# Three opening tiles rebuilt: a convolution summed on TensorE, halves copied by ScalarE and VectorE, GpSimd relieved, a growing lookahead

## What is computed

```python
# attention part: x (4, 4096, 192), weight_gen (4, 4096, 8 heads, 7 taps)
w = exp(weight_gen - max(weight_gen, -1)); w = w / (sum(w, -1) + 1e-9)
y[b, s, h, g] = sum_k w[b, s, h, k] * x_pad[b, s + k, h, g]      # 6 zeros of padding ahead
# layer: 16384 tokens, d_model 192, d_ff 1536
xn = y / sqrt(mean(y * y, -1) + 1e-6) * rms_g
g = xn @ w_gate; out = (g * sigmoid(g) * (xn @ w_val)) @ w_out
```

## Time and profile before

| quantity | us |
|---|---|
| median of 3 runs | 1334.81 |
| lowest, highest | 1332.93, 1335.38 |
| the profiled execution | 1334.78 |
| its span on the core | 1333.0 |

### The profile page before, as it was taken

How to read it: one execution, slowest core, us unless ns; L and a number is a source line. 1 busy time by engine, 2 the same in 40 slices (tenths; PEclk the granted TensorE clock), 3 DMA queues, 4 the chain that set the end, 5 groups by cost and what they waited for, 6 DMA issues and landing times.

```text
span 1333.0 us, 33644 instructions
## 1 busy us (share of the span) xinstructions
PE 1280.2 (96%) x13524; PEld 1230.0 (92%) x13524; DVE 995.2 (75%) x1438; ACT 662.8 (50%) x1427; POOL 97.1 (7%) x104
## 2 busy tenths in 40 slices
PE   3797899999999999999999999999999999999998
PEld 3686789999988889999999999999999999999998
DVE  6777867877777777777777777777777777777653
ACT  4364464455554455554445555445555544555543
POOL 7701200000000000000000000000000000000000
PEclk9798899999999999999999999999999999999999
DMA  9121111122112212212112211211221211121010
GB/s 306 35 67 25 50 58 55 37 67 67 49 60 64 57 37 66 66 43 66 54 40 63 66 58 51 66 55 37 66 66 43 66 55 52 52 66 34 16 37 13
DMA packets 20101, 77.69 MB, mean 58 GB/s; under 512 B 3215, under 2 KB 5007, under 8 KB 19854
## 3 DMA queue, kind: packets, MB, share of 16 engines
q1 hardware_dynamic: 19982, 75.83, 19.0%
HBM read 38.07 MB, written 12.58 MB: 38 GB/s over the span
## 4 chain that ended last, share of the span: by engine, by line
PE 91%; DVE 3%; ACT 2%; issue 2%; DMA 1%; POOL 0%; SPq 0%; POOLq 0%
PE up_ps L619 59%; PE out_ps L650 24%; PE out_ps L654 7%; DVE h L545 1%; DMA xT<-xT 1%; DVE prod L201 1%; PE up_ps L587 1%; DVE y L203 1%; ACT silu L422 0%; DVE tap_max L522 0%; ACT taps L403 0%; DVE h_lo L565 0%; ACT xn L386 0%; PE up_ps L591 0%; DMA taps<-in_weight_gen 0%
## 5 line engine op out<-in xcount | busy, mean ns | idle before, releaser
L619 PE MATMUL up_ps<-xT,w_hi 64*128 64x512 f32 x4608 | 823.3, 395 | 14.3 <-DVE h L545 6.8
L619 PEld LDWEIGHTS up_ps<-xT,w_hi 64*128 64x128 f32 x4608 | 540.2, 186 | 44.8 <-DMA xT<-xT 7.5
L619 PE MATMUL up_ps<-xT,w_lo 64*128 64x512 f32 x2304 | 521.8, 394 | 0.0
L650 PE MATMUL out_ps<-wo,h_hi 64*128 64x384 f32 x3072 | 468.4, 356 | 14.3 <-DVE h L545 12.6
L545 DVE TENSOR_TENSOR h<-up_ps,silu 128x512 f32<-128x512 f32 x384 | 264.9, 690 | 248.8 <-ACT silu L422 248.7
L654 PE MATMUL out_ps<-wo,h_lo 64*128 64x192 f32 x3072 | 433.6, 248 | 0.0
L429 ACT ACTIVATE h_hi<-h 128x512 fp32r<-128x512 f32 x384 | 242.7, 632 | 355.0 <-DVE h L545 355.0
L650 PEld LDWEIGHTS out_ps<-wo,h_hi 64*128 64x128 f32 x3072 | 370.7, 186 | 18.4 <-issue 14.9
L654 PEld LDWEIGHTS out_ps<-wo,h_lo 64*128 64x128 f32 x3072 | 372.9, 189 | 2.1
L422 ACT ACTIVATE silu<-up_ps 128x512 f32<-128x512 f32 x384 | 228.7, 596 | 274.9 <-PE up_ps L619 270.7
L619 PEld LDWEIGHTS up_ps<-xT,w_lo 64*128 64x128 f32 x2304 | 282.0, 186 | 12.9
(11 more groups left out here) (43 smaller groups left out, 315.2 us busy)
## 6 DMA issues: line engine op xcount, KB each, us to landing
x_buf<-in_x SPq DMA_DIRECT2D x30, 960.0 KB, 4.6
xT<-xT SPq DMA_DIRECT2D x96, 256.0 KB, 3.8
result<-last SPq DMA_DIRECT2D x32, 384.0 KB, 2.3
taps<-in_weight_gen SPq DMA_DIRECT2D x1, 3248.0 KB, 19.4
raw<-in_moe_w_gate SPq DMA_DIRECT2D x3, 384.0 KB, 6.4
raw<-in_moe_w_val SPq DMA_DIRECT2D x3, 384.0 KB, 7.5
last<-in_moe_w_out SPq DMA_DIRECT2D x1, 1152.0 KB, 12.4
x_first<-in_x SPq DMA_DIRECT2D x2, 384.0 KB, 4.9
```

Source lines behind the costliest of these rows:

```text
L619: mm = nc.tensor.matmul(ps[:, banks, :], w[rows, s, cols], xT[rows, t, s, part, :], start=(s == 0 and n == 0), stop=ends)
L650: nc.tensor.matmul(out_ps[:, j, 0:2 * D], h_hi[rows, g % HB, cols], wo[rows, g, :, :].rearrange("p a d -> p (a d)"), start=(g == 0 and k < ...
```

## The change

- **DMA order.** SyncE issues the taps of tile 0, x of tile 0, then per slot: gate weights, a piece of gains, value weights, a piece of gains (six pieces now). Taps and x for the following tiles come after. The halo is now loaded by four DMAs that ScalarE issues, after GpSimd has zeroed all of it.
- **Tile 0's convolution.** VectorE makes seven products without waits in between, in seven buffers, and adds the last two. TensorE sums the six through the identity matrix into the output banks (`sum_first`). ScalarE squares and scales from PSUM.
- **Tile 0's and tile 1's input.** ScalarE and VectorE each scale two of the four token columns. ScalarE makes the second copies of the high parts (`x_high_moved`) and VectorE those of the low parts (`x_low_moved`); no DMA copies for these tiles. Tile 1 is no longer transposed inside tile 0: tile 0 ends with its own last projection, then the squares, scalings, transposes and copies of tile 1 follow.
- **GpSimd** convolves nothing and subtracts nothing. Tile 1 is convolved by VectorE in blocks 4 to 10 of tile 0.
- **Lookahead.** In tile 0 VectorE works on tile 1's convolution only. In tiles 1 and 2 it does 27 and 24 steps for tiles 2, 3 and 4 (`steps_1`, `steps_2`), and from tile 3 on it is two tiles ahead as before.
- **The other taps.** They begin with tile 4. The pieces are 5, 11 and 12 tiles; maximum and subtraction are both on VectorE, in tile 1 (blocks 8 and 10), tile 4 and tile 5 (blocks 3 and 7), the exponentials on ScalarE in tile 2 (block 1), tiles 4 and 5 (block 9).
- **Turns.** `turn_after` is 11, 9, 7 for tiles 0, 1, 2 and 5 after them. ScalarE's squares and scalings for the next tile stand at blocks 7 and 8 in tile 1, at 3, 4 and 5, 6 in tile 2, at 0 to 3 later.
- **Weights.** `w_low` and the `wo` pair are done in halves, part of them inside tile 0.
- **Warm turns.** 50 before the sum of tile 0 and 30 after it.

The diff, cut to its core:

```diff
-    FIRST = 3
+    FIRST = 4
-            return 9 if isinstance(T, int) and T == 0 else 5
+            return {0: 11, 1: 9, 2: 7}.get(T, 5) if isinstance(T, int) else 5
-        cuts = [FIRST, 8, 20, TILES]
+        cuts = [FIRST, 9, 20, TILES]
+        def moves(t, part):
+            low, high = slice(0, DB), slice(DB, P)
+            return tuple((xT[to, t, slot, part, :], xT[of, t, source, part, :].bitcast(F32))
+                         for to, of, slot, source in ((low, high, 1, 0), (high, low, 1, 0), (high, low, 2, 2)))
-        WARM_TURNS = 84
+        WARM_TURNS, KEEP_TURNS = 50, 30
...
+            load_taps(0)
+            load_first(0)
+            for s in range(SLOTS):
+                load_w(s, 0, w_gate)
+                load_gains(s, 0)
+                load_w(s, 1, w_val)
+                load_gains(s, 1)
+            load_taps(1)
+            load_first(1)
...
+            act.wait_ge(halo_zeroed, 1)
+            for b in range(B):
+                p = b * (S // TOK)
+                act.dma_start(x_first[p + 1:p + S // TOK, 0:PAD, :],
+                              x_d[p:p + S // TOK - 1, TOK - PAD:TOK, :]).then_inc(halo_loaded, 16)
             first_exps(0)
-            act.wait_ge(gains_loaded, 80)
+            act.wait_ge(gains_loaded, 96)
...
+            def x_high_moved(T, t, banks):
+                act.wait_ge(xT_done, T + 1)
+                main, rest = 3 * T + 1, 3 * T + 3
+                nc.scalar.activation(main_to(t, 0), main_of(banks), ACT.Copy).then_inc(x_hi_done, 1)
+                if T == 1:
+                    for odd in range(2):
+                        nc.scalar.activation(rest_to(t, 0, odd), rest_of(banks, odd), ACT.Copy).then_inc(x_hi_done, 1)
+                act.wait_ge(x_hi_done, main)
+                for to, of in moves(t, 0)[0:2]:
+                    nc.scalar.activation(to, of, ACT.Copy).then_inc(hi_moved, 1)
...
+                squares_at, scales_at = {9: ((7,), (8,)), 7: ((3, 4), (5, 6)), 5: ((0, 1), (2, 3))}.get(xf, ((), ()))
...
+                if first:
+                    square(1, 1, range(J))
+                    scale(1, 1, range(J // 2))
+                    x_high_moved(1, 1, pair(0, xf + 1))
...
+            for k in range(K):
+                nc.vector.tensor_tensor(heads(first_prods[k]), heads(flat(x_first[:, k:k + J, :])),
+                                        tap_w[:, :, k].unsqueeze(2).to_broadcast([P, J * H, G]), ALU.mult).then_inc(first_mix, 1)
+            dve.wait_ge(first_mix, NORM + K)
+            nc.vector.tensor_tensor(first_prods[K - 2], first_prods[K - 2], first_prods[K - 1], ALU.add).then_inc(first_mix, 1)
+            for s in range(SLOTS):
+                w_low(0, s)
+            less_max(1)
+            scale_rest(0, 0)
+            w_low(1, 0)
+            x_low_moved(0, 0, 1)
...
+            seconds = [0, 0, 0, 0, 2, 2, 2, 1, 2, 2, 2, 0]
+            steps_taps = [2, 2, 2, 0, 2, 2, 2, 0, 2, 1, 1, 1]
+            steps_1 = [(2, 5), (2, 2), (2, 2), (2, 2), (2, 2), (2, 2), (2, 2), (3, 4), (3, 2), (3, 1), (3, 2), (3, 1)]
+            steps_2 = [(3, 2), (3, 2), (3, 3), (4, 4), (4, 2), (4, 2), (4, 2), (4, 1), (4, 2), (4, 2), (4, 1), (4, 1)]
...
+                    for b in range(2):
+                        cols = slice(b * 2 * D, (b + 1) * 2 * D)
+                        mm = nc.tensor.matmul(out_ps[:, b, 0:2 * D], ident[:], first_prods[k][:, cols],
+                                              start=(k == 0), stop=(k == K - 2))
...
+                if first:
+                    project(T, FB - 2)
+                    pe.wait_ge(silu_done, xf)
+                    pe.wait_ge(h_done, xf)
+                    pe.wait_ge(xn_done, 4 * J)
+                    turn_x(1, 1, pair(0, xf + 1))
...
             for _ in range(WARM_TURNS):
+                nc.tensor.transpose(up_ps[:, 0, 0, 0:P], ident[:], ident[:])
+            sum_first()
+            for _ in range(KEEP_TURNS):
                 nc.tensor.transpose(up_ps[:, 0, 0, 0:P], ident[:], ident[:])
```

More of the change, by code:

```diff
@@ L263, in turn @@
                         store(T - 1, (t + 1) % 2)
-                    if not (last and t == 1):
+                    if not (first and t == 0 or last and t == 1):
                         copy_halves(T + 1, 1 - t)
@@ L422, in tile @@
                     nc.scalar.activation(silu[:, f % 2, :], gate_ps[:, b, :], ACT.Silu).then_inc(silu_done, 1)
-                    if f == xf and not last:
+                    if first and f in (0, 4):
+                        wo_high(f // 4)
+                    if f == xf and not (first or last):
                         x_high(T + 1, 1 - t, pair(t, xf + 1))
@@ L490, in first_step, with w_low, wo_low @@
                 dve.wait_ge(first_mix, at + 1)
+            def w_low(n, s):
+                cols = slice(n * F // 2, (n + 1) * F // 2)
+                dve.wait_ge(w_hi_done, s + 1)
+                nc.vector.scalar_tensor_tensor(out=w_lo[:, s, cols], in0=raw[:, s, cols], scalar=gains[:, s:s + 1],
+                                               in1=w_hi[:, s, cols].bitcast(F32), op0=ALU.mult,
+                                               op1=ALU.subtract).then_inc(w_lo_done, 1)
+            def wo_low(n):
+                fs = slice(n * FB // 2, (n + 1) * FB // 2)
+                dve.wait_ge(w_hi_done, SLOTS + 1 + n)
+                nc.vector.tensor_tensor(wo[:, fs, 1, :], raw_out[:, fs, :], wo[:, fs, 0, :].bitcast(F32),
+                                        ALU.subtract).then_inc(wo_lo_done, 1)
             dve.wait_ge(first_exp, 1)
@@ L505, in _ @@
-            for s in range(SLOTS):
-                if s == SLOTS - 1:
-                    x_low(0, 0, 1)
-                dve.wait_ge(w_hi_done, s + 1)
-                nc.vector.scalar_tensor_tensor(out=w_lo[:, s, :], in0=raw[:, s, :], scalar=gains[:, s:s + 1],
-                                               in1=w_hi[:, s, :].bitcast(F32), op0=ALU.mult,
-                                               op1=ALU.subtract).then_inc(w_lo_done, 1)
-            def wo_low():
-                dve.wait_ge(w_hi_done, SLOTS + 1)
-                nc.vector.tensor_tensor(wo[:, :, 1, :], raw_out, wo[:, :, 0, :].bitcast(F32),
-                                        ALU.subtract).then_inc(w_lo_done, 1)
+            dve.wait_ge(xfirst_loaded[0], 16)
@@ L566, in tile @@
                                             ALU.subtract).then_inc(h_lo_done, 1)
+                    if f == max_at:
+                        rest_maxima(piece)
+                    if f == subtract_at:
+                        rest_subtract(piece)
+                if first:
+                    scale_rest(1, 1)
+                    x_low_moved(1, 1, pair(0, xf + 1))
             tile(0, 0, 0, first=True)
@@ L571, in _ @@
             tile(3, 1, 1)
-            with dve.Fori(2, TILES // 2 - 1) as i:
+            tile(4, 0, 2)
+            tile(5, 1, 2)
+            dve.wait_ge(rest_exp, len(pieces))
+            with dve.Fori(3, TILES // 2 - 1) as i:
                 tile(2 * i, 0, i)
@@ L675, in tile @@
                     if f == 0:
-                        if not first:
+                        if T > 1:
                             project(T - 1, FB - 2)
@@ L683, in tile @@
                         else:
-                            pe.wait_ge(w_lo_done, SLOTS + 1)
-                    if f + 1 == xf and not last:
+                            pe.wait_ge(wo_lo_done, 1)
+                    if first and f == 8:
+                        pe.wait_ge(wo_lo_done, 2)
+                    if f + 1 == xf and not (first or last):
                         pe.wait_ge(silu_done, FB * T + xf)
```

301 lines of the change are left out of this document (175 added, 126 removed).

## The result

| | median, us | lowest, highest | against the runs beside it |
|---|---|---|---|
| before | 1335.10 | 1332.93, 1336.02 | |
| changed | 1352.15 | 1351.23, 1353.72 | 1.0126, 95% interval 1.0112 to 1.0140 |

The change makes the kernel 1.3% slower, 17 us, where 15 us less were forecast. The profiled execution took 1351.23 us with a span of 1349.4, against 1334.78 and 1333.0 before.

A forecast was written before the change was run, and what follows sets the result against it. TensorE, busy 96% of the span, bounds the kernel; only the opening and three tiles' excess can give. Opening 32.4 plus six tiles (48.0, 43.6, 43.5, 39.6, 42.1, 42.1) makes 291.3 against 306.41: 15.1 less, 1319.5 us; range 1306 to 1328.

The forecast's parts named there:

- Step 1, the halo: Opening: tile 0's products can start near 7.5 us instead of 8.46; the halo may be late by up to 1.
- The rival for the slow side: Clock: gaps of tile 0 keep TensorE at half speed; 24 us of such work gives 1343 us; chance 0.04.
- The halo is late: Opening: float32 sum on the path at 1.5 us a matmul, or halo late: 5 us more, 1325; chance 0.12.
- I am wrong if the first mark stands above 38: Sign of failure in the opening: tile 0's first Silu, forecast near 32.4 us, comes after 38.
- Step 2, the products: Tile 0's convolution on VectorE: seven products and one addition take 7.5 us, done between 15 and 16 instead of 23.13.
- Step 3, the sum: Opening, TensorE's sum of six products: 0.42 us a matmul, up to 1.0 still covered; sum stands near 16.5 us.
- Step 4, the gains: Opening: gains end behind the last weights, near 17 us instead of 19.29; squares until 23.5; 3.5 us less if gains pass.
- Step 5, GpSimd: Opening: GpSimd's two operations done by 25.7 us, 3.3 earlier than before; bounds 1 and 4.3 us after the squares.
- Steps 6 and 7: Scaling split, 1.15 instead of 2.24 us, first product near 28.6; engine copies, first Silu 32.4, 11.3 earlier, bounds 15.5 and 5.5.
- Tile 0: Mark 0 to mark 1: 39.5 us plus losses of 1.6 clock, 1.5 VectorE, 3.9 turn, 1.5 clock: 48.0 against 44.7.
- Tiles 1 and 2: Tile 1: 37.3+6.3 = 43.6 us against 49.7; tile 2: 39.3+4.2 = 43.5 against 50.4.
- Tiles 4 and 5: 42.1 us each: maximum delays the low split by 2.0, exponential costs 0.5 to 0.8; bounds 0 to 5 of loss each.

The follow-up runs named there:

- e1: Changed kernel with each of its four halo DMAs of 31 partitions cut into one of 16 and one of 15: 1326.02 us, ratio 0.9924.
- e2: Changed kernel with its four halo DMAs of 31 partitions issued by SyncE behind the first x, instead of by ScalarE: 1344.84 us, single execution.
- e3: Kernel before with its two halo DMAs of 112 and 15 partitions replaced by a single one of 127: 1359.32 us, single execution.
- e4: As e1, with the six gains DMAs issued ahead of the six weights: 1321.94 us, ratio 0.9894.
- e5: As e4, but SyncE issues the halo as 112 and 15 partitions behind the first taps, and GpSimd zeroes four rows afterwards: 1319.64 us, ratio 0.9880.
- e8: As e5, with the gains behind the weights of slot 0 and VectorE zeroing two of the four rows: 1318.20 us, ratio 0.9872.
- e9: As e8, with the other taps in six pieces of 4 or 5 tiles instead of three: 1313.92 us, ratio 0.9836.
- e6: Kernel before with the subtraction of the maximum for all three pieces moved from GpSimd to VectorE: 1324.36 us, ratio 0.9927.
- e7: As e4, with SyncE's DMAs copying the halves for tiles 0 and 1 instead of ScalarE and VectorE: 1339.58 us, single execution.
- e10: As e8, but VectorE adds all seven products and TensorE only moves the finished sum by one matmul pair: 1324.50 us, single execution.

## Why the prediction was wrong, point by point

- **Step 1, the halo.** This is the step that failed. It said "this may be late by up to 1 us", a bound taken from nothing but the order of issue. It was late by 36 us: the products start at 44.08 instead of 7.5 to 8.5. The kernel before has no DMA of a prime partition count, its halo being cut in 112 and 15, and I changed that cut without asking what it does. Had the bound been asked for, 124 packets of 4.6 KB one after the other would have been the upper end. e1, e2 and e3 show the cause from three sides. Some 5 of the 36 us vanish on the way to the first Silu, mostly since `w_hi` has long been made by then; 31 are left.
- **The rival for the slow side** was the clock, at 1343. The clock did fall in the long wait (0.50 from 14.5 to 48.6 us), but as a result, and TensorE had little to do in it. "The halo is late" stood among the rivals, at 5 us, without a mechanism. "I am wrong if the first mark stands above 38" was the sign that came.
- **Step 2, the products.** Right: 0.88 us from start to start, seven of them and the addition in 7.2 us, for 7.5.
- **Step 3, the sum.** The price was 0.42 to 1.0 us for a matmul of 384 columns in float32 and is 0.65 at full clock. The cover held as long as the clock did. In the changed kernel TensorE had idled for 34 us, the sum took from 45.09 to 54.8, and the squares started 3.0 us after the end of VectorE's last addition; it is 3.3 us in e1 and 4.1 in e4. The prediction had counted the clock only behind the sum, not in front of it.
- **Step 4, the gains.** Right in kind: e1 to e4 brings `w_hi` from 20.04 to 12.39 at the first slot, so the gains did wait. The 3.5 us that this was priced at aren't shown by the 4.1 between the two runs, as the squares waited for the sum in both. The weights don't come 2 us sooner than before, however: 19.48 for the last in e4 against 19.29. And the upper bound of 15.5 us in step 7 was added up wrongly: 11.3 and 3.5 are 14.8.
- **Step 5, GpSimd.** Right: 1.3 us for both operations instead of 4.3, and VectorE is done by then, as the step had it.
- **Steps 6 and 7.** From `inv_rms` to the first Silu the changed kernel takes 6.4 us, where 6.7 had been worked out. Before, it was 14.7. The copies cost 0.63 on ScalarE and 0.43 on VectorE.
- **With the halo mended.** e1 is the changed kernel with nothing else mended: opening 36.0 for 32.4, time 1326.0 for 1319.5. That is in the stated range and 6.5 us above the forecast: 3.6 in the opening, 1.6 in the six tiles, and the rest behind them or between the profiled execution and the median. The halo there still lands at 16.2 instead of 8.5. e4, e5 and e8 (1321.9, 1319.6, 1318.2) change the DMA order as well, so that they come near 1319.5 is no proof of the working.
- **Tile 0** was 2.5 us shorter than forecast. `h_lo` was 1.68 late, for 1.5. The turn of tile 1 left 0.79 us of wait before its first product and 0.8 more inside the block, for 3.9. The clock was back at full at 48.6, before the first product, so the 1.6 us charged at the start weren't lost. It fell once behind the wait for `h_lo`, from 99.8 to 103.2 us, as forecast.
- **Tiles 1 and 2** came out to 0.1 us in their sums, in tile 1 by luck. TensorE's waits there are 0.89, 0.86 and 2.36 us, forecast 0.9, 1.2 and 3.4, and no wait of 0.8 us for the DMA copies is seen: 4.1 us instead of 6.3. In their place the granted clock fell to 0.50 from 140.8 to 144.2 us, right behind the 2.36 us wait, while TensorE was busy throughout; that costs up to 1.7 us, and the prediction had no term for it in this tile. In tile 2 the waits are 0.65, 1.12 and 1.61 us, forecast 0.6, 1.3 and 2.1 (which add up to 4.0 and not to the 4.2 that was put in).
- **Tiles 4 and 5** cost 4.1 and 4.6 us, forecast 2.8. The exponential was mis-sized: 1.4 and 1.83 us of wait for 0.5 to 0.8. The maximum and the low split behind it came to 1.5 and 1.7 us, for 2.0. Some 1.1 to 1.2 us of each tile stand in no wait of TensorE above 0.15 us, and what they are stays open. e9 shows that the excess hangs on the length of the single instructions and not on the table loads, of which it has more.

**How the gain divides.** Part by part, from the runs: the subtraction off GpSimd about 10 us, in the old frame (e6); the copies by the engines 17.6 us, in the new opening (e7, a single execution, against e4); the sum on TensorE 6 us (e10, a single execution, against e8). They don't add up, since each was taken out of another frame. The open turn of tile 1 and the larger tiles 4 and 5 give some of it back: e6, with the old handling of tiles, has 252.2 us for its first six tiles, and the changed kernel 259.1.

## What to carry to other kernels

Before a DMA is added or cut anew, look at its partition count: 31 and 127 each put the whole DMA on one DMA engine here, and what stood behind it in the queue waited as well. 31 cut into 16 and 15, and 127 into 112 and 15, did not. An operation that no row of the trace shows in its shape needs an upper bound from a mechanism, not from goodwill, and that holds most for the one on which all else waits. And if a large, well reasoned change comes out slower by tens of microseconds, undo nothing before the chain of waits is read: here one line of it named the fault, and cutting four DMAs in two gave back 26 us.

## What the runs showed of the hardware

- A DMA of 31 partitions ran on one of the DMA engines: the four of them had 124 packets of 4.6 KB from 4.6 to 43.0 us, most of which took 0.18 to 0.36 us. One of 127 partitions did the same (e3, 30 packets fewer than the cut of 112 and 15).
- SyncE's queue was slowed with it, though the halo stood in ScalarE's: ScalarE waited for the six gains DMAs until 28.9 us in the changed kernel and until 20.0 in e1, and SyncE's issue of two x loads took 28.1 us against 9.0. That SyncE was held by a full queue is my reading; no view shows it.
- A float32 matmul of 128x128 by 384 columns takes 0.65 us at full clock, and a pair 2.93 instead of 1.29 us at a granted clock of 0.50, after 13 us of idling (e10). It took 2.89 us after 2.9 us of idling in e5, where the clock was at 0.50 too, and 1.56 after 0.8 us in e8 at full clock.
- ScalarE needs 5.0 us for eight DMA issues (e1), in which it does nothing else.
